# Delta-rule attention inside a three-stage kernel: the order of one phase's steps on four engines, and its loops over chunks written out

## The reference

```python
# stage 1, for each of 4 batches x 8 heads, 768 positions, head size 48
k_n = k / (norm(k) + 1e-06)
for t in range(S):
    y[:, :, t] = einsum('bhd,bhde->bhe', q[:, :, t], state)
    v_old = einsum('bhde,bhd->bhe', state, kt)
    state = state + bt * einsum('bhd,bhe->bhde', kt, vt - v_old)
# stage 2: x = y, as 3072 x 384
h = x @ w_in; r = maximum(h, 0); g = s * (r * r) + b; x = g @ w_out
# stage 3: each row goes to the expert (of 8) that its logits choose
out[mask] = gate_w[mask, None] * (maximum(x[mask] @ w1[e], 0) @ w2[e])
```

## Time and profile before

| | us |
|---|---|
| median of 3 runs (lowest, highest) | 1160.63 (1160.08, 1163.29) |
| the profiled execution's own time | 1159.56 |
| its span, first to last instruction | 1157.8 |
| stage 1 (to the start of stage 2) | 450.7 |
| stage 2 | 427.3 |
| stage 3 | 279.8 |

### The profile page before, as it was taken

One profiled execution on the slowest core, in us unless ns is written; L12 is line 12 of the kernel. 1 busy time (PEld: TensorE's weight loads), 2 busy tenths in 40 slices (PEclk: granted clock), 3 DMA queues, 4 the chain that ended last, 5 costly groups with the idle time before them and its releaser, 6 DMA issues. The chain is left out here.

```text
span 1157.8 us, 28648 instructions
## 1 busy us (share of the span) xinstructions
PE 1044.8 (90%) x10998; PEld 898.0 (78%) x10998; DVE 640.2 (55%) x1051; ACT 496.4 (43%) x1007; POOL 403.1 (35%) x333
## 2 busy tenths in 40 slices
PE   3899898998989985999999999999994699999997
PEld 2788787888878874788787878878782588988886
DVE  5676576776777753645344343534435555445555
ACT  3564455655555643444233333423331434333433
POOL 5656446456546431005023050501302523212223
PEclk9798789988889987999999999999997799999999
DMA  9223333223330004401010010100000813444423
GB/s 149 61 52 65 69 75 63 45 58 71 68 76 16 16 16 134 154 1 55 0 55 0 0 54 0 54 0 27 0 0 27 273 64 123 140 163 163 149 93 112
DMA packets 135378, 79.38 MB, mean 69 GB/s; under 512 B 78414, under 2 KB 126038, under 8 KB 135286
## 3 DMA queue, kind: packets, MB, share of 16 engines
q1 hardware_dynamic: 132886, 73.27, 23.4%
q10 hardware_dynamic: 2400, 4.72, 1.1%
HBM read 63.03 MB, written 14.94 MB: 67 GB/s over the span
## 5 line engine op out<-in xcount | busy, mean ns | idle before, releaser
L1170 DVE SCALAR_TENSOR_TENSOR m_act_r<-m_act_r,m_sb_col 128x512 f32<-128x512 f32 x96 | 84.0, 875 | 144.2 <-ACT m_act_r L1097 144.2
L1488 POOL TENSOR_TENSOR e_w_lo<-e_w_raw,e_w_hi 128x384 fp32r<-128x384 f32 x64 | 72.6, 1144 | 177.2 <-ACT e_w_hi L1510 177.2
L1097 ACT ACTIVATE m_act_r<-m_hid 128x512 f32<-128x512 f32 x96 | 57.0, 594 | 142.1 <-PE m_hid L1215 140.2
L1173 DVE SCALAR_TENSOR_TENSOR m_g_lo<-m_act_r,m_sb_col,m_g_hi 128x512 fp32r<-128x512 f32 x96 | 75.5, 786 | 76.0 <-ACT m_g_hi L1100 76.0
L1215 PE MATMUL m_hid<-m_x_hi,m_w_hi 128*128 128x512 f32 x288 | 113.1, 393 | 4.3 <-DVE m_x_lo L1158 4.3
L1100 ACT ACTIVATE m_g_hi<-m_act_r,m_sb_col 128x512 fp32r<-128x512 f32 x96 | 69.5, 724 | 102.6 <-DVE m_act_r L1170 102.6
L1215 PE MATMUL m_out<-m_g_hi,m_w_hi 128*128 128x512 f32 x288 | 112.9, 392 | 0.5 <-DVE m_g_lo L1173 0.3
L1045 POOL TENSOR_TENSOR m_sq<-m_x_f 128x512 f32<-128x512 f32 x15 | 15.2, 1041 | 282.0 <-ACT m_x_f L1107 282.0
L1215 PE MATMUL m_hid<-m_x_lo,m_w_hi 128*128 128x512 f32 x288 | 112.9, 392 | 0.0
L1215 PE MATMUL m_hid<-m_x_hi,m_w_lo 128*128 128x512 f32 x288 | 112.8, 392 | 0.0
L1215 PE MATMUL m_out<-m_g_hi,m_w_lo 128*128 128x512 f32 x288 | 112.2, 390 | 0.0
(11 more groups left out here) (225 smaller groups left out, 2674.4 us busy)
## 6 DMA issues: line engine op xcount, KB each, us to landing
e_w_raw<-in_moe_w_dram SPq DMA_DIRECT2D x64, 384.0 KB, 7.1
a_b_rows<-in_beta_dram SPq DMA_DIRECT2D x48, 128.0 KB, 3.6
e_x_raw<-x2T_scratch SPq DMA_DIRECT2D x8, 768.0 KB, 4.7
out_dram<-e_acc SPq DMA_DIRECT2D x7, 768.0 KB, 3.5
a_k_raw<-in_k_dram SPq DMA_DIRECT2D x24, 192.0 KB, 3.8
a_q_raw<-in_q_dram SPq DMA_DIRECT2D x48, 96.0 KB, 3.0
a_v_raw<-in_v_dram SPq DMA_DIRECT2D x24, 192.0 KB, 3.6
xT_scratch<-a_y_T SPq DMA_DIRECT2D x48, 96.0 KB, 2.0
```

The source lines that it names most:

```text
L1097: nc.scalar.activation(act_r[:, f % RING, :], hid[f % RING][:, :], ACT.Relu).then_inc(s["relu_ready"], 1)
L1170: nc.vector.scalar_tensor_tensor(out=r, in0=r, scalar=sb_col[:, 0:1], in1=r, op0=ALU.mult, op1=ALU.mult).then_inc(s["sq_ready"], 1)
L1173: nc.vector.scalar_tensor_tensor(out=g_lo[:, f % RING, :], in0=r, scalar=sb_col[:, 1:2], in1=f32(g_hi[:, f % RING, :]), op0=ALU.add, op1=A ...
L1488: nc.gpsimd.tensor_tensor(w1_lo[:, :, c], w1_raw[:, :, c], f32(w1_hi[:, :, c]), ALU.subtract).then_inc(s["w1_lo_ready"], 1)
```

## The change

Two things change, both in stage 1, and no instruction that computes is added or removed.

First, `Fori` loops over chunks become Python loops on all five engines, so phases 2 to 11 are written out in the program. Waits whose count was worked out in registers from c become waits on constants.

Second, the lists `phase` of POOL, ACT, DVE and PE have another order.

SP, and in the same way gp, act, dve and pe:

```diff
-            with sp.Fori(0, NC - 2) as c:
+            for c in range(NC - 2):
...
-            with pe.Fori(0, NC - 1) as c:
+            for c in range(NC - 1):
```

The list of POOL, whole:

```diff
             def phase(prep, solve, following):
+                keys_to_transpose(prep, 1)
+                masked_scores(solve, 1)
+                scaled_keys(prep, 1)
+                masked_scores(solve, 0)
+                keys_to_keep(prep, 1)
+                unit_diagonal(solve, 1)
                 square(following)
-                masked_scores(solve, 0)
-                keys_to_transpose(prep, 1)
-                scaled_keys(prep, 0)
+                scaled_values(prep)
+                low_part(prep, 1)
+                keys_to_transpose(following, 0)
                 keys_to_keep(prep, 0)
-                keys_to_keep(prep, 1)
-                scaled_keys(prep, 1)
-                low_part(prep, 1)
-                scaled_values(prep)
                 low_part(prep, 0)
                 unit_diagonal(prep, 0)
-                keys_to_transpose(following, 0)
-                masked_scores(solve, 1)
-                unit_diagonal(prep, 1)
+                scaled_keys(following, 0)
```

The list of DVE, cut:

```diff
             def phase(prep, solve, following):
-                masked(prep, 0, 0, 1)
-                masked(prep, 0, 1, 0)
-                masked(prep, 0, 1, 1)
-                sum_squares(following)
                 residual(solve, 0, 1)
-                small_blocks(prep, 0)
                 masked(prep, 1, 0, 0)
                 masked(prep, 1, 0, 1)
                 masked(prep, 1, 1, 0)
                 masked(prep, 1, 1, 1)
+                small_blocks(prep, 0)
                 residual(solve, 1, 0)
...
                 small_out(prep, 1)
+                take_beta(prep)
                 off_blocks(prep, 1)
...
                 small_out(prep, 4)
+                sum_squares(following)
+                residual(solve, 1, 3)
+                small_out(prep, 5)
                 small_spread(prep, 0)
...
-                take_beta(following)
...
+                residual(prep, 0, 0)
                 large_spread(prep, 0)
-                new_state(solve, 1)
-                new_state(solve, 0)
-                residual(prep, 0, 0)
                 large_spread(prep, 1)
                 masked(following, 0, 0, 0)
+                masked(following, 0, 0, 1)
+                masked(following, 0, 1, 0)
+                masked(following, 0, 1, 1)
+                new_state(solve, 1)
```

The list of PE, cut (ACT's list follows it: each copy of a result moves with the matmuls that make it, and `scores(prep, 1, 0, 1)` opens its phase):

```diff
             def phase(prep, solve, following):
+                key_products(prep, 1, 0)
+                key_products(prep, 1, 1)
                 correction(solve, 0, 1)
...
-                small_step(prep, 0, 2)
                 small_step(prep, 1, 0)
                 gather(solve, 0, 2)
+                off_transposes(prep, 0)
+                small_step(prep, 0, 2)
+                small_step(prep, 1, 1)
+                correction(solve, 1, 1)
+                correction(solve, 0, 3)
                 small_step(prep, 0, 3)
-                correction(solve, 1, 1)
-                small_step(prep, 1, 1)
-                off_transposes(prep, 0)
...
+                state_change(solve, 0)
+                new_output(solve, 0)
+                across_blocks(prep, 1, 1)
                 correction(solve, 1, 4)
...
-                key_products(following, 1, 0)
-                key_products(following, 1, 1)
```

More of the change, by code:

```diff
@@ L436, in phase @@
                 update_out(solve, 1)
-                result_out(solve, 0)
-                transposed(following, 0)
+                transposed(following, 1)
                 large_out(prep, 0, 3)
                 large_out(prep, 1, 3)
-                transposed(following, 1)
                 transposed(following, 2)
                 transposed(following, 3)
+                delta_out(prep, 0, 0)
                 scores(following, 0, 0, 1)
@@ L446, in phase @@
                 scores(following, 0, 1, 1)
-                delta_out(prep, 0, 0)
+                scores(following, 0, 1, 0)
                 high_part(following, 0)
-                scores(following, 0, 1, 0)
                 result_out(solve, 1)
-                scores(following, 1, 0, 1)
             phase(None, None, (0, 0))
             phase((0, 0), None, (1, 0))
-            with act.Fori(0, NC - 1) as c:
+            for c in range(NC - 1):
                 phase((1, c), (0, c), (0, c + 1))
@@ L868, in phase @@
+                gather(solve, 1, 1)
                 small_step(prep, 0, 4)
-                small_step(prep, 1, 2)
-                correction(solve, 0, 3)
-                gather(solve, 1, 1)
-                small_step(prep, 0, 5)
                 small_step(prep, 1, 3)
                 gather(solve, 0, 3)
-                small_step(prep, 0, 6)
+                correction(solve, 1, 2)
                 small_step(prep, 1, 4)
-                correction(solve, 1, 2)
+                small_step(prep, 0, 5)
@@ L878, in phase @@
                 off_transposes(prep, 1)
                 correction(solve, 0, 4)
+                gather(solve, 1, 2)
+                small_step(prep, 0, 6)
                 small_step(prep, 1, 5)
-                gather(solve, 1, 2)
+                gather(solve, 0, 4)
+                sum_of_deltas(solve, 0)
+                small_step(prep, 1, 6)
+                correction(solve, 1, 3)
                 large_step(prep, 0, 0)
-                small_step(prep, 1, 6)
-                gather(solve, 0, 4)
+                old_output(solve, 0)
@@ L885, in phase @@
                 across_blocks(prep, 0, 0)
-                correction(solve, 1, 3)
-                sum_of_deltas(solve, 0)
                 large_step(prep, 1, 0)
+                correction(solve, 0, 5)
                 gather(solve, 1, 3)
-                old_output(solve, 0)
+                large_step(prep, 0, 1)
                 across_blocks(prep, 1, 0)
+                transposes(following, 0)
+                across_blocks(prep, 0, 1)
+                large_step(prep, 1, 1)
+                state_change(solve, 0)
@@ L892, in phase @@
+                new_output(solve, 0)
+                across_blocks(prep, 1, 1)
                 correction(solve, 1, 4)
-                large_step(prep, 0, 1)
-                transposes(following, 0)
-                large_step(prep, 1, 1)
+                large_step(prep, 0, 2)
+                transposes(following, 1)
+                large_step(prep, 1, 2)
                 gather(solve, 1, 4)
-                correction(solve, 0, 5)
-                across_blocks(prep, 0, 1)
-                across_blocks(prep, 1, 1)
+                across_blocks(prep, 0, 2)
@@ L900, in phase @@
+                across_blocks(prep, 1, 2)
                 sum_of_deltas(solve, 1)
-                large_step(prep, 0, 2)
-                large_step(prep, 1, 2)
-                new_output(solve, 0)
-                across_blocks(prep, 0, 2)
+                large_step(prep, 1, 3)
                 correction(solve, 1, 5)
-                across_blocks(prep, 1, 2)
-                transposes(following, 1)
+                large_step(prep, 0, 3)
+                state_read(prep, 0)
                 old_output(solve, 1)
-                large_step(prep, 0, 3)
```

48 lines of the change are left out of this document (24 added, 24 removed).

## The result

The changed kernel takes 1094.67 us (median of 4 runs, 1093.93 to 1095.15) where the kernel before takes 1161.86 on the same chip. The ratio is 0.9415, with a 95% interval of 0.9396 to 0.9434: 67 us faster. A second set of four runs on another occasion gave 1093.68 (1091.47 to 1094.78), ratio 0.9417 [0.9368, 0.9466].

What follows compares the result with a forecast made beforehand. PE's own stream was taken as the bound, with only stalls and clock to win. Branches, masks less new waits, and clock gave 42 us over ten phases, the ends 3: 1159.6 to 1114.6, forecast 1115 us, range 1102 to 1131.

Steps and rivals of the forecast that it cites:

- the clock term: Ten phases of stage 1: PE's mean granted clock rises from about 0.87 to 0.92, worth 1.2 us a phase.
- PE's two waits: Each phase: small_step waiting for DVE's small_blocks (7.6 us over seven), correction waiting for residual (12.5 us over ten).
- fourth rival: Stage 1: the stalls go and the clock stays full, 1098 to 1102 us; chance 0.08.
- three rows of waits: PE in ten phases: issue 11.8 us, correction for residual 12.5, small_step for small_blocks 7.6; together 31.9 us.
- best case of 29.0 a phase: Ten phases without waits for DVE and at full clock: 290 us, 1098 with the ends.
- New waits: PE in the changed order: 0.5 us a phase charged for waits that arise anew.
- Branches: PE's four taken loop branches, after phases 3, 5, 7 and 9, vanish: 14.5 us saved.
- Masks: DVE's 16-bit masks stand until POOL's running instruction ends; keeping POOL idle saves 2.0 us of PE waits a phase.
- Ends: Outside the ten phases: phase 12 gains 2.5, phase 13 loses 0.5, phases 0 and 1 gain about 1; together 3 us less.
- The wait did not move to another place: First rival: masks freed but POOL's later work makes PE wait as long; 1140 to 1147 us, chance 0.12.
- POOL is not late at the end of the phase: Second rival: scaled_keys(following, 0), behind everything in POOL's list, comes late; 1160 us and above, chance 0.02.
- Straight code is fetched in time: Third rival claimed the opposite: fetch misses of 3.3 to 4.0 us; some 13 use up the gain, chance 0.02.

Runs made afterwards that it cites:

- freed masks, old order of PE: Kernel before with loops written out; only take_beta moved before off_blocks(prep, 1) on DVE and scaled_values ahead of low_part(prep, 1) on POOL: 1113.45 us.
- clock full (filler): Kernel before with loops written out, plus 18 unread 128-column matmuls ahead of each of the two PE steps that wait for DVE: 1132.76 us.
- POOL's pause: keys_to_transpose(following, 0) between the two low_part: added to the old order with freed masks 1111.6 us; taken from the changed kernel (with keys_to_keep moved too) 1109.7 us.
- The first half of the new order: Old order with freed masks, but PE, ACT and DVE in the new order in the phase's first half: 1125.11 us; with POOL's pause added, 1113.05 us.
- the early copy: Changed kernel with DVE's take_beta(prep) moved from the fourth mask to the phase's second place: 1128.76 us; with 14 filler matmuls, 1112.64 us.

## Why the prediction was wrong in size

**The step that failed** is the clock term of the sum: "With most stalls gone I take the mean from 0.87 or so to 0.92, worth 1.2 us." The clock came to 1.00 in all ten phases. Splitting the ten phases into the time in which PE is busy and the time in which it is idle shows what this was worth:

| ten phases, us | PE busy | PE idle | sum |
|---|---|---|---|
| before | 314.9 | 34.1 | 349.0 |
| forecast | 302.9 | 4.6 | 307.5 |
| freed masks, old order of PE | 291.4 | 12.4 | 303.8 |
| changed kernel | 284.0 | 2.4 | 286.4 |

The row of the forecast takes its 12 us of clock from the busy time, and its 14.5 + 20 - 5 from the idle time. The idle time came out 2 us from the forecast. The other 19 of the missing 21 us are busy time, which fell by 30.9 us where the forecast had 12.

Of these 30.9, 23.5 are there while PE's list is still in the old order: 314.9 - 291.4, at a clock of 1.00. They go with the clock phase by phase. PE is busy 31.7 us at 0.85, 31.2 at 0.90 and 30.1 at 0.95, and 29.1 at 1.00 with the masks freed, always with some 665 matmuls. So the clock term was sized at 12 us, and by this split it was worth 23.5, about twice as much. The direction was right, and so was the cause: the clock is full as soon as PE's two waits are filled, or the masks freed. The prediction's own price, 1.2 us for 0.05, would have given about 3 us a phase for the way from 0.87 to 1.00. It had this case as its fourth rival, 1098 to 1102 with a chance of 0.08, though the earlier trace rows put the fall and the stalls into the same phases.

**The order of PE's steps** had no term at all: "so PE's own stream is the bound, and only its stalls and its clock can give time back". In idle time that reading was right for the kernel before, whose three rows of waits leave 349.0 - 314.9 - 31.9 = 2.2 us. But at the same clock of 1.00 PE's busy time falls by a further 7.4 us between the kernel of the freed masks and the changed one. The mean time of one matmul is the same in both (183 ns for `correction`, 166 for `small_step`), so this lies in how matmuls follow each other inside stretches that count as busy. That is why the best case of 29.0 a phase was no bound: 28.6 was measured.

**New waits** were charged with 5 us and did not come: 2.4 us of idle time are left, as much as lay outside the named waits before.

The kernels also make a ladder over the ten phases. Each difference holds for the order in which the changes are made here.

| ten phases, us | after this step | gain | forecast |
|---|---|---|---|
| before | 349.0 | | |
| loops written out | 336.1 | 12.9 | 14.5 |
| and clock full (filler) | 320.8 | 15.3 | 12 |
| and masks freed (no filler) | 303.8 | 17.0 | 20 less 5 of new waits |
| and the rest of the order | 286.4 | 17.4 | 0 |
| sum | | 62.6 | 41.5 |

**Branches:** near, 12.9 against 14.5 in the old order. PE's waits for issue had been 11.8, and with them gone the wait for `small_blocks` stands in ten phases instead of seven. In the new order PE's loop is worth 24, since each turn stalls for longer and takes the clock down where it would be full.

**Masks:** right in place and mechanism. The step of 17.0 also takes the filler out, whose own time hides part of the clock's gain in the step above it, and it brings the new wait for `small_spread`. All four lines now have a median of 0.68 or 0.69 us; `small_spread`, for which 0.5 had been allowed, is clean in the ten phases.

**The last step, 17.4 us,** is 10.0 of idle time and 7.4 of busy time. The 12.4 us of idle time that it starts from are mostly not in the kernel before: 6.7 are the wait for `small_spread`.

What makes these 17 us is shown in part. POOL's pause is necessary: without it the changed kernel loses 14.0 of them. Given to the old order it yields 1.5, though there it frees the mask only in part. The first half of the new order adds nothing to it either (303.5, with two phases at a clock of 0.95). So the rest needs what these kernels lack, together with the pause: the second half of PE's, ACT's and DVE's lists (the key products at the start of the phase, state and output steps between the large steps), DVE's `masked` and `sum_squares` in their new places, and the rest of POOL's new list. Which of these moves carries it was not tried and stays open.

**Ends:** forecast 3 less, measured 2.7, but not in the parts forecast. Phase 12 went from 30.1 to 26.1, 4.0 less where 2.5 were forecast. The first `correction` of phase 2 went from 50.6 to 51.8, 1.2 later where 1 less was forecast; a second profiled execution of the changed kernel has it at 51.6. What follows phase 12 stayed at 21.0 and 21.1.

**Rivals.** The wait did not move to another place: PE's waits have one row of 0.4 us. POOL is not late at the end of the phase. Straight code is fetched in time: PE has that one wait for issue of 0.4 us, DVE and ACT have none in the ten phases, and POOL's are at `scaled_values`, which `take_beta` releases. Nor is more fetched. The two instruction queues moved 1.39 MB before and 1.30 MB after. Before, then after:

```profile
q8 instruction: 78, 1.28, 0.5%
q14 instruction: 14, 0.11, 0.0%
```

```profile
q8 instruction: 68, 1.11, 0.4%
q14 instruction: 23, 0.19, 0.1%
```

## What to carry to other kernels

Split an engine's time into busy and idle before you add up what a change is worth. Here the idle part was forecast to 2 us, and nearly the whole miss was in the busy part. Busy time is no floor: with the same matmuls it moved with the clock, from 31.5 to 29.1 us a phase, and with the order of the steps, to 28.4. A best case that is worked out by taking the named waits away is then no bound.

Where the clock falls after PE's waits, price every wait twice, once as a wait and once as clock. Read the price of the clock from phases with the same work, and carry a case at full clock with its whole price. A few matmuls that nothing reads, put into the wait, show in one run that the clock is part of it.

Where instructions on DVE and POOL hold each other up, what a collision costs depends also on the room behind the mask: taking the pause away cost 14.0 us in one order, and giving it, with the mask freed in part, yielded 1.5 in another. A wait that keeps POOL idle at the right moment can be worth more than POOL's time.

## What the hardware showed that was not expected

Added matmuls made the kernel faster: 36 more a phase, 15.3 us less over ten phases, at 1.00 instead of about 0.90 of the clock. The Trainium skill (TensorE: Matmul & The Clock Gate, section "What's actually happening") has the throttled clock as the default and activity as what releases it; the trace agrees.

Not every wait of PE takes the clock down. With the two `low_part` together PE waits 1.0 us in every phase for `small_spread`, and the clock stays at 1.00. With the early copy it waits 1.2 us a phase in two pieces, and the clock is 0.85 to 0.95. No run shows what makes the difference.

PE's branch back costs more when the loop's body begins with the key products: 17.2 us over four turns, longest 4.7, where the loop before had 11.8, longest 3.3. No run shows why.

The loops of the other four engines cost nothing that can be seen in the old order: written out on all five, they gave 12.2 us, where PE's waits for issue alone had been 11.8. That is read from the sizes; no run has the loops of those four alone.
